# Causal mask in an attention and gated-MLP kernel: a rank-one mask matmul becomes an add inside VectorE's row maximum

## The reference

```python
scores = scale * np.matmul(q, k.transpose(0, 1, 3, 2))     # scale = 1/8
mask = block_i >= block_j                                  # blocks of 64 positions
scores = np.where(mask, scores, -1000000000.0)
scores = scores - np.max(scores, axis=-1, keepdims=True)
attn = np.exp(scores)
attn = attn / (np.sum(attn, axis=-1, keepdims=True) + 1e-09)
out = np.matmul(attn, v)
...
h = x @ w_in;  g = h * relu6(h + 3) / 6;       x = g @ w_out    # first layer
h = x @ w_in2; g = h * np.tanh(softplus(h));   y = g @ w_out2   # second layer
```

## Time and profile before

| what | value |
|---|---|
| runs | 993.1, 993.25, 990.79 us; median 993.1 |
| the profiled execution | 992.28 us, its span 990.5 us |
| TensorE clock granted over the span | 0.998 |
| busy over the span | PE 97%, PEld 87%, DVE 77%, ACT 65%, POOL 45% |
| mask matmuls (L750) | 128, 308 ns in the median, first at 8.6 us, last at 204.7 us |
| row maxima (L1337) | 160, first at 9.5 us, last at 207.6 us |

### The profile page before, as it was taken

How to read it: one execution, slowest core, us unless ns; L and a number is a source line. 1 busy time by engine, 2 the same in 40 slices (tenths; PEclk the granted TensorE clock), 3 DMA queues, 4 the chain that set the end, 5 groups by cost and what they waited for, 6 DMA issues and landing times.

```text
span 990.5 us, 17992 instructions
## 1 busy us (share of the span) xinstructions
PE 962.7 (97%) x6132; PEld 859.8 (87%) x6132; DVE 758.6 (77%) x1443; ACT 644.6 (65%) x1429; POOL 446.9 (45%) x412
## 2 busy tenths in 40 slices
PE   6999899999999999999999999999999999999998
PEld 5888898999888898898889888899889898898896
DVE  5888898978686766769798786876877877777654
ACT  6888788856454554544446556777777777776663
POOL 6776899867765576969676680000000000000000
PEclk9999999999999999999999999999999999999999
DMA  7778667754789978587967545646645645465255
GB/s 163 212 188 253 169 175 203 189 154 145 236 274 326 301 264 285 182 288 273 330 226 259 220 149 177 238 151 219 237 162 211 234 177 196 170 231 201 90 189 194
DMA packets 81914, 211.49 MB, mean 214 GB/s; under 512 B 12320, under 2 KB 19104, under 8 KB 81824
## 3 DMA queue, kind: packets, MB, share of 16 engines
q1 hardware_dynamic: 81744, 210.06, 65.1%
q10 hardware_dynamic: 80, 0.29, 0.1%
HBM read 170.39 MB, written 39.92 MB: 212 GB/s over the span
## 4 chain that ended last, share of the span: by engine, by line
PE 77%; DVE 6%; ACT 2%; DMA 2%; issue 1%; SPq 1%; ACTq 0%; DVEq 0%
PE psum L962 35%; PE psum L845 11%; PE psum L847 11%; PE psum L846 11%; PE psum L795 3%; PE psum L774 3%; PE psum L752 2%; PE psum L754 1%; DVE ebuf L1514 1%; PE psum L750 1%; DVE glo L1520 1%; DVE xlo L1449 1%; DMA ext_d<-ext_made 1%; DMA o_d<-staged 1%; DVE ext_made L1420 1%
## 5 line engine op out<-in xcount | busy, mean ns | idle before, releaser
L962 PE MATMUL psum<-ghi,osplit 128*128 128x512 f32 (+1 forms) x640 | 215.9, 371 | 0.4 <-POOL osplit L1767 0.4
L845 PE MATMUL psum<-xhi,whi 128*128 128x256 f32 (+1 forms) x640 | 187.4, 293 | 2.2 <-ACT snap L1163 2.0
L847 PE MATMUL psum<-xhi,wlo 128*128 128x256 f32 (+1 forms) x640 | 186.8, 292 | 0.0
L846 PE MATMUL psum<-xlo,whi 128*128 128x256 f32 (+1 forms) x640 | 186.6, 292 | 0.0
L962 PE MATMUL psum<-osplit,ghi 128*128 128x512 f32 x576 | 180.9, 395 | 1.1 <-DVE glo L1520 0.9
L1520 DVE SCALAR_TENSOR_TENSOR glo<-ebuf,ghi 128x512 fp32r<-128x512 f32 x144 | 124.0, 861 | 24.8 <-ACT ghi L1211 16.8
L845 PEld LDWEIGHTS psum<-xhi,whi 128*128 128x128 f32 x640 | 120.8, 189 | 15.2 <-ACT snap L1163 3.6
L1767 POOL TENSOR_TENSOR osplit<-oraw,osplit 128x512 fp32r<-128x512 f32 x80 | 115.2, 1442 | 38.4 <-ACT osplit L1130 34.2
L962 PEld LDWEIGHTS psum<-ghi,osplit 128*128 128x128 f32 x640 | 117.9, 189 | 16.4 <-issue 0.6
L1211 ACT ACTIVATE ghi<-ebuf 128x512 fp32r<-128x512 f32 x144 | 90.2, 627 | 62.9 <-DVE ebuf L1514 34.4
L846 PEld LDWEIGHTS psum<-xlo,whi 128*128 128x128 f32 x640 | 120.8, 189 | 10.7
(11 more groups left out here) (113 smaller groups left out, 2250.8 us busy)
## 6 DMA issues: line engine op xcount, KB each, us to landing
ext<-ext_d SPq DMA_DIRECT2D x56, 768.0 KB, 4.3
osplit<-o_d SPq DMA_DIRECT2D x80, 512.0 KB, 5.6
oraw<-in_w_out SPq DMA_DIRECT2D x80, 256.0 KB, 5.6
qkin<-in_qk SPq DMA_DIRECT2D x63, 288.0 KB, 4.4
wraw<-in_w_in SPq DMA_DIRECT2D x32, 512.0 KB, 5.6
ext_d<-ext_made SPq DMA_DIRECT2D x32, 384.0 KB, 5.5
attn_t<-ostage SPq DMA_DIRECT2D x64, 144.0 KB, 3.2
o_d<-staged SPq DMA_DIRECT2D x32, 256.0 KB, 5.2
```

The lines of the kernel that those rows point to most:

```text
L845: pe.matmul(dst, hi, xh, start=(start and cc == 0), stop=False, skip_group_check=True)
L846: pe.matmul(dst, hi, xl, start=False, stop=False, skip_group_check=True)
L847: last = pe.matmul(dst, lo, xh, start=False, stop=(stop and cc == 1), skip_group_check=True)
L962: last = pe.matmul(bank(Y_BANK + c, n), stat, mov, start=(first and m == 0), stop=(final and m == 2), skip_group_check=True)
```

## The change

The mask becomes an SBUF tile `mask` of one number per block of 64 columns (128 rows by 9), zero but for -1e30 in the last column of the first 64 rows. `row_max` becomes one `tensor_tensor_reduce`: it reads the scores from PSUM and the mask from SBUF (each mask number spread over 64 columns by a stride of zero), adds them, multiplies by -1/8, writes the result to `prob`, and keeps the row's minimum. The exponential reads `prob` in SBUF and writes to the same place, with scale -1; for row tile 4 it now runs over 640 columns, the pad included, so the pad's exponentials are also in the row sums of that tile. The mask matmuls are gone; `scores` starts its accumulation with the `khi` product, and waits on `max_ready`, the count of finished row maxima, where it waited on `exp_done`.

```diff
-            mask_rows = ab("mask_rows", [P, P], F32R)
-            mask_val = ab("mask_val", [P, P], F32R)
+            mask = ab("mask", [P, SEQ // DH], F32)
...
         def score_tile(n, i):
-            s, b = n % 2, score_banks(n, i)
-            if i < 4:
-                return bank(b, PW[i]), prob[s][:, POFF[i]:POFF[i] + PW[i]]
-            return (bank(b, 2 * BANK).rearrange("p (a k) -> p a k", a=2)[:, :, 0:SEQ // 2],
-                    prob[s][:, POFF[4]:POFF[4] + SEQ].rearrange("p (a k) -> p a k", a=2))
+            b, groups = score_banks(n, i), (2 if i == 4 else PW[i] // DH)
+            src = (bank(b, PW[i]).rearrange("p (a k) -> p a k", a=groups) if i < 4 else
+                   bank(b, 2 * BANK).rearrange("p (a k) -> p a k", a=2)[:, :, 0:SEQ // 2])
+            dst = prob[n % 2][:, POFF[i]:POFF[i] + min(PW[i], SEQ)].rearrange("p (a k) -> p a k", a=groups)
+            added = mask[:, SEQ // DH - groups:] if i < 4 else mask[:, 0:2]
+            return src, dst, added.unsqueeze(2).broadcast_to(list(src.shape))
...
                 if i < 4 and n > 0:
-                    pe.wait_ge(exp_done, ST * (n - 1) + min(i + 3, ST))
+                    pe.wait_ge(max_ready, ST * (n - 1) + min(i + 3, ST))
                 if i == 4:
-                    pe.wait_ge(exp_done, ST * n + 2)
+                    pe.wait_ge(max_ready, ST * n + 2)
...
-                    if i < 4:
-                        pe.matmul(bank(pb, P, PW[i] - P), mask_rows[:, :], mask_val[:, :],
-                                  start=True, stop=False, skip_group_check=True)
-                    pe.matmul(bank(pb, w), q_tile, khi[s][:, k0:k0 + w], start=(i == 4), stop=False,
-                              skip_group_check=True)
-                    last = pe.matmul(bank(pb, w), q_tile, klo[s][:, k0:k0 + w], start=False, stop=True,
-                                     skip_group_check=True)
+                    pe.matmul(bank(pb, w), q_tile, khi[s][:, k0:k0 + w], start=True, stop=False)
+                    last = pe.matmul(bank(pb, w), q_tile, klo[s][:, k0:k0 + w], start=False, stop=True)
...
-                src, dst = score_tile(n, i)
+                dst = prob[s][:, POFF[i]:POFF[i] + PW[i]]
                 col = i * HEADS + n % HEADS
-                nc.scalar.activation(dst, src, ACT.Exp, bias=negmax[s][:, i:i + 1], scale=SCALE,
+                nc.scalar.activation(dst, dst, ACT.Exp, bias=negmax[s][:, i:i + 1], scale=-1.0,
                                      accum_out=rowsum[n // HEADS % 2][:, col:col + 1]).then_inc(exp_done, 1)
...
+                if n == 0 and i == 0:
+                    dve.wait_ge(consts_ready, 2)
                 dve.wait_ge(scores_ready, ST * n + i + 1)
                 if i == 0 and n >= 2:
                     dve.wait_ge(p_transposed, PT * (n - 1))
-                src, dst = score_tile(n, i)
-                nc.vector.tensor_scalar(dst, src, -SCALE, None, ALU.mult, ALU.min,
-                                        accum_out=negmax[s][:, i:i + 1]).then_inc(max_ready, 1)
+                src, dst, added = score_tile(n, i)
+                nc.vector.tensor_tensor_reduce(dst, src, added, -SCALE, -MASKED, ALU.add, ALU.min,
+                                               negmax[s][:, i:i + 1]).then_inc(max_ready, 1)
```

More of the change, by code:

```diff
@@ L994, in attention_step @@
                     h_part_step(0, 4, 9)
-            pe.wait_ge(consts_ready, 3)
+            pe.wait_ge(consts_ready, 2)
             pe.wait_ge(pads_zero, 6)
@@ L1788, in next_x @@
                             split_x_lo(blk, cc, i)
-            raw_rows, raw_val = oraw[0][:, 0:P], oraw[0][:, P:2 * P]
-            nc.gpsimd.memset(oraw[0][:, 0:P + DH], 0.0).then_inc(memset_done, 1)
-            nc.gpsimd.memset(oraw[0][:, P + DH:2 * P], MASKED).then_inc(memset_done, 1)
+            nc.gpsimd.memset(mask[:, :], 0.0).then_inc(memset_done, 1)
             nc.gpsimd.memset(ident[:, :], 0.0).then_inc(memset_done, 1)
@@ L1796, in _ @@
             nc.gpsimd.memset(one, 1.0).then_inc(memset_done, 1)
-            pool.wait_ge(memset_done, 5)
-            nc.gpsimd.memset(raw_rows[0:1, 0:DH], 1.0).then_inc(memset_done, 1)
+            pool.wait_ge(memset_done, 4)
+            nc.gpsimd.memset(mask[0:DH, SEQ // DH - 1:], MASKED).then_inc(consts_ready, 1)
             nc.gpsimd.affine_select(out=ident[:, :], in_=ident[:, :], compare_op=ALU.not_equal, fill=1.0,
                                     base=0, pattern=[[-1, P]], channel_multiplier=1).then_inc(consts_ready, 1)
-            nc.gpsimd.tensor_copy(mask_val[:, :], raw_val).then_inc(consts_ready, 1)
-            pool.wait_ge(memset_done, 6)
-            nc.gpsimd.tensor_copy(mask_rows[:, :], raw_rows).then_inc(consts_ready, 1)
             for n in range(FIRST, NHEAD):
```

## The result

The changed kernel takes 982.87 us (median of 4 runs, 982.52 to 985.06) against 992.72 us for the kernel before (4 runs, 990.79 to 993.25): ratio 0.9909, interval 0.9889 to 0.9929, so 0.7 to 1.1% faster. Its profiled execution took 982.52 us with a span of 980.7; before it was 992.28 and 990.5, so 9.8 us less.

The account below looks back on a forecast made before the run. TensorE was taken to set attention's pace, with VectorE, ScalarE and GpSimd close behind. Gains of 3.6 + 1.8 + 1.1 + 3.4 + 0.5 + 0.3 = 10.7 us gave 982.4 us, range 979.0 to 993.5 less half a us at the low end.

Parts of the forecast that it names:

- The instruction's price: VectorE's new row maximum: costs what the old one did, or 10 ns less; nearest row 680 ns at 512 columns.
- The bound from two SBUF operands: VectorE's new maximum: if the mask stream is held up as two SBUF operands are, 0.17 us more in the mean.
- The exponential: ScalarE: reading SBUF instead of PSUM costs 35 ns more each, taking a head from 5.13 to 5.36 us.
- Ordinary heads: Heads without extra work, 3 + 7 of them: 5.43 us each, 0.36 gained a head, 3.6 us in all.
- In ordinary heads it hardly waited there.: TensorE at score banks: earlier release gains about 0.4 us only in the four heads behind ScalarE's weight split.
- The second stretch: Heads 4 to 13: gains of 0.4 behind ScalarE's split, 0.25 behind VectorE's, 0.36 in ordinary heads; 3.4 us.
- The fourth and last stretches: Heads 16 to 21, held by GpSimd at 5.58 us, gain 1.8 us; heads 25 to 31, ordinary, gain 2.5.
- the third rival: TensorE gets faster but GpSimd's ring of loads keeps the 5.8 us pace; 3 us gained, 990 us; chance 0.13.
- the three signs: Forecast wrong if VectorE's starts spread over 0.16 us after a maximum, TensorE awaits `q_lo` at tile 0, or layers await weights.
- The fifth stretch: Heads 22 to 24: ScalarE at 5.64 + 0.23 = 5.87 us, so 5.95 a head; 1.1 us gained.
- The start and the stall: First head's score tiles gain 0.3 us; heads 14 and 15, whose 2.65 us stall stays, gain 0.5.
- the second case: VectorE sets the pace, 5.55 to 5.6 us a head, through 0.08 us more a maximum; 987 us; chance 0.17.

Follow-up runs that it names:

- e9: Changed kernel with an unread reduction of 64 score columns ahead of each of the five row maxima; 987.90 us, ratio 0.9950.
- e10: Changed kernel with an unread reduction of 128 score columns ahead of each of the five row maxima; 994.49 us, ratio 1.0023.
- e4: Changed kernel with the widest exponential over 576 columns instead of 640, the pad left out; 983.16 us, ratio 0.9913.
- e2: Changed kernel with a matmul of zeros where each mask matmul stood, early release of score banks kept; 990.23 us, ratio 0.9975.
- e1: Changed kernel with score banks released only after the exponential, as before the change; 988.15 us, ratio 0.9963.
- e3: Kernel before with the mask matmuls taken out and nothing in their place, exponential still reading PSUM; 985.89 us, ratio 0.9935.
- e7: Changed kernel with SyncE issuing the load of the values before that of queries and keys; 981.71 us, ratio 0.9881.
- e8: Changed kernel with GpSimd's three low halves of x in steps 22, 24, 26 instead of 22, 23, 24; 984.49 us, ratio 0.9907.
- e11: Changed kernel with the values loaded before queries and keys, and all early work on x one head later; 979.40 us, ratio 0.9867.
- e5: Changed kernel with a memset of 32 columns, read by nobody, ahead of each of the five row maxima; 985.14 us, ratio 0.9916.

## Why the prediction was right, point by point

*The instruction's price.* Right, and the step that mattered most: 690 ns at 512 columns before and after, taken from the nearest row, that with one operand in PSUM and one in SBUF. The bound from two SBUF operands (0.17 us more) lies between the doses of e9 and e10 and so would have brought the kernel about level with the one before. The Trainium skill's rule in "SBUF — State Buffer", section "Who interferes with whom", by which an instruction with one SBUF input keeps out of GpSimd's way, agrees with that: GpSimd was busy for 34.01 of the 39.13 us of the last stretch, and the mean stayed at 690.

*The exponential.* Right within 3 ns by listed durations at 512 and 384 columns (32 and 33 ns more, 35 forecast), and a little too small by starts. The listed durations grew by only 12 ns at 128 columns (386 to 398) and 4 at 256 (499 to 503). But what holds ScalarE is the distance from the exponential's start to the next row's, the read of its accumulator. Before, at 128 columns:

```profile
186.11 0.39 ACT L1036 ACTIVATE prob<-psum,small 128x128 f32<-128x128 f32 x1
186.36 0.23 ACT L1036 ACTIVATION_READ_ACCUMULATOR prob<-psum,small 128x1 f32 x1
```

In the changed kernel:

```profile
25.45 0.40 ACT L1031 ACTIVATE prob<-prob,small 128x128 f32<-128x128 f32 x1
...
25.75 0.20 ACT L1031 ACTIVATION_READ_ACCUMULATOR prob<-prob,small 128x1 f32 x1
```

In the mean over the 32 of each width this distance grew from 251 to 293 ns at 128 columns, from 356 to 401 at 256, from 465 to 507 at 384 and from 569 to 613 at 512, so by 42 to 45 ns at each. The Trainium skill, "VectorE: DVE Perf Modes", section "The TRN2 errata — SBUF-src ops pay a fixed extra latency per instruction", states 224 cycles from SBUF against 172 from PSUM, by the prediction's estimate 43 ns; the trace agrees, read by starts. Where the exponential lies on the ring it costs more than the sum had; in the changed kernel's ordinary head the widest one does not lie there (e4).

*Ordinary heads.* 5.41 us against 5.43. The mask matmul's price of 0.11 us is borne out by no window of its own, but e2's ordinary head, with matmuls of zeros back in place and TensorE busy throughout, is 0.35 us longer: 0.09 for each of four. The spare time of VectorE, 5.0 us of its own work, came out at 4.97 and 4.98.

*"In ordinary heads it hardly waited there."* This is the step that was wrong, though it cost the sum nothing, and in that the number was lucky. It was true of the trace before, where TensorE's own work covered the wait for the exponential; with that work gone the wait would have come out in every ordinary head, as in e1. The early release was priced at 0.4 us in each of four heads, and is worth 0.29 in each ordinary head (5.70 to 5.41) once the masks are gone. Behind ScalarE's split the forecast 0.40 came out, but not from the release alone: that gave 0.05 (e2), the masks' going alone 0.22 (e3). The sum came out since it took for granted what the release brought, a TensorE that waits for nothing. A price for half of the change would have missed by that much. The reading that TensorE sets the pace because it is busy for all of a head does not hold by itself: in e3 it is so too, and 0.16 us of its head are a wait.

*The second stretch* was undersized, 4.18 against 3.4. Heads 4, 7 and 13 gained the 0.40 that was worked out, heads 6, 9 and 12 less than their 0.36 (0.28, 0.06 and 0.28). Heads 5, 8 and 11, behind VectorE's split, gained 0.67 where 0.25 stood, nearly all of it from the release (e2), which the prediction had not counted there.

*The fourth and last stretches* were oversized: 0.86 against 1.8, and 1.32 against 2.5 (seven heads at 0.36). Here the third rival held in part. TensorE idles in front of tile 0 for `q_lo`, one of the three signs that the prediction named. In heads 19 to 21 the cause is the load of the values, as e7 shows. In the last stretch what is missing lies in heads 25 to 27, 17.72 us where the sum had 3 x 5.43 = 16.29. TensorE's timeline has two of the waits:

```profile
163.06 0.33 PE L749 MATMUL psum<-khi,qs 128*128 128x128 f32 x1 [0.58 <-POOL qs L1648]
...
169.28 0.33 PE L749 MATMUL psum<-khi,qs 128*128 128x128 f32 x1 [0.68 <-POOL qs L1648]
```

e7, in which no values are late here, has the same two waits, 0.58 and 0.68 us, and e8 moved them along with GpSimd's low halves of x: here it is GpSimd's own work. A pace of 5.8 us had hidden that; one of 5.4 does not. Why head 27 is long too, at 5.78 us and without such a wait, stays open.

*The fifth stretch*, 0.82 against 1.1: the prediction put its bound on ScalarE. ScalarE's busy time came near the forecast (17.39/3 = 5.80 us a head against 5.87), and in head 24, of 5.67 us, it is busy throughout. Head 22 took 6.19. In it TensorE waits 0.74 us for `q_lo`, up to 145.38 us, 4.3 us after GpSimd began another piece of work on x (L1732, 1.29 us). In e11, where that piece comes one head later, the wait does too (0.68 us in head 23), and head 22 takes 5.78. Head 23, of 6.25 us, is open: ScalarE's split of x stands in it as well, and no run tells the two engines apart there.

*The start and the stall* were undersized by 0.5 and 0.4 us. Neither says anything. The first widest exponential started at 14.10 and 14.31 us in the two profiles of the changed kernel, and anywhere from 13.98 to 15.03 over all profiles. Head 14 took 8.29 and 9.99 us in the same two profiles.

The sum of the stretches of attention was forecast at 10.7 us and came out at 10.3: two terms too large by 2.1 together against smaller ones in the other direction, so that the time came out 0.5 us from the forecast is in part luck. The layers gave 0.5 back; the profile shows no cause, and it lies within what executions differ by (781.2 to 783.2 us over all profiles). VectorE as the pace, the second case, came near only behind VectorE's splits: in the changed kernel's head 5 it is busy for all but 0.01 us, though e4's shorter exponential took 0.07 us off such heads, so it does not set them alone.

```profile
36.40:42.36 5.96, 4.90 (x38) 4.30 (x38) 5.95 (x16) 5.32 (x17) 5.43 (x6) 1.00 0.82 211
```

## What to carry to other kernels

When several engines stand close to the pace, take the busy time off the one at the top and ask which ring stands right under it; here the masks alone were worth 0.22 us in an ordinary head, the earlier release with the masks' work in place 0.03, and the whole change 0.38. A busy share of 100% can hide a wait; the distance between two neighbouring starts, held against the same place in another run, shows it. Work that is moved to an engine in an instruction that it runs anyway can be free, and whether it is, is read from the nearest row with the same places of operands; the spare time of that engine, counted by starts, says how wrong that row may be. A faster pace lays bare the loads that the old one covered, and the side work of an engine, so look at the order in which a queue issues loads, and at that work, once the pace has moved.

## What was not expected of the hardware

Listed durations and starts tell different stories of ScalarE. By the list the price of SBUF depends on the width (32 and 33 ns at 512 and 384 columns, 12 at 128, 4 at 256), and the read of the accumulator became shorter (216 ns before, 195 after, over 160 of each). By starts the exponential costs 42 to 45 ns more at each of these widths, and the read holds its successor for about 0.1 us in both kernels. On VectorE a memset of 32 columns, listed at 0.09 us, starts together with the instruction behind it (both at 29.81 us in e5), while a reduction of 64 columns of PSUM holds it by 0.13.
